# 256-token tiles at both ends of a fused token-mixing and two-layer kernel, with softmax by tile and weight pieces by order of need

## What is computed

```python
# x: (2, 4096, 192), weight_gen: (2, 4096, 8 heads, 7)
w = softmax(weight_gen, axis=-1)                      # 7 mixing weights for each token and head
x_pad = concat([zeros(B, 6, D), x], axis=1)           # causal window of 7 tokens
out[b, s, h, :] = sum_k w[b, s, h, k] * x_pad[b, s + k, h, :]
x = out.reshape(8192, 192)
x = (sigmoid(x @ w_gate) * (x @ w_val)) @ w_out1      # 192 -> 1536 -> 192
h = x @ w_in                                          # 192 -> 2048
P = a0 + a1*h + a2*h**2 + a3*h**3
Q = 1 + |b0|*|h| + |b1|*h**2
return (P / (Q + 1e-6)) @ w_out2                      # 2048 -> 192
```

## Time and profile before

| | before |
|---|---|
| median of three runs | 1456.27 us |
| the profiled execution, its own time | 1456.45 us |
| its span | 1454.7 us |
| PE busy | 1375.1 us (95%), 7040 matmuls |
| weight loads on PE | 1224.0 us (84%) |
| DVE busy | 1221.6 us (84%) |
| ACT busy | 1047.2 us (72%) |
| POOL busy | 356.3 us (24%) |
| moved by DMA | 36.22 MB, 25 GB/s in the mean |

### The profile page before, as it was taken

One profiled execution on the slowest core, in us unless ns is written; L12 is line 12 of the kernel. 1 busy time (PEld: TensorE's weight loads), 2 busy tenths in 40 slices (PEclk: granted clock), 3 DMA queues, 4 the chain that ended last, 5 costly groups with the idle time before them and its releaser, 6 DMA issues.

```text
span 1454.7 us, 18169 instructions
## 1 busy us (share of the span) xinstructions
PE 1375.1 (95%) x7040; PEld 1224.0 (84%) x7040; DVE 1221.6 (84%) x1327; ACT 1047.2 (72%) x1357; POOL 356.3 (24%) x204
## 2 busy tenths in 40 slices
PE   2679999999999999999999999999999999999876
PEld 1568889888989988898988889898888988898765
DVE  6554989888988988898898889889888988888898
ACT  3325877877777787777778777877877787787774
POOL 0534123231413323141332314132231423200000
PEclk9889999999999999999999999999999999999999
DMA  8410001001010100101010010101001010000000
GB/s 208 117 75 1 31 1 42 0 1 42 1 42 0 42 1 1 42 1 42 1 42 1 0 42 0 42 1 42 1 1 41 1 42 1 11 1 11 0 11 11
DMA packets 13103, 36.22 MB, mean 25 GB/s; under 512 B 1240, under 2 KB 6872, under 8 KB 12760
## 3 DMA queue, kind: packets, MB, share of 16 engines
q1 hardware_dynamic: 12952, 35.05, 8.2%
q0 software_dynamic: 64, 0.00, 0.0%
HBM read 27.16 MB, written 7.90 MB: 24 GB/s over the span
## 4 chain that ended last, share of the span: by engine, by line
PE 88%; DVE 8%; ACT 2%; issue 1%; DMA 1%; SPq 0%; ACTq 0%; DVEq 0%
PE ring L284 48%; PE acc L312 37%; DVE work L630 1%; DVE work L639 1%; DVE work L623 1%; PE ring L339 1%; DVE work L609 1%; PE ring L342 1%; DVE work L603 1%; DMA window<-in_x_dram 1%; DVE work L616 1%; DVE mixed L530 0%; DVE prod L525 0%; DVE in_w L566 0%; ACT work L433 0%
## 5 line engine op out<-in xcount | busy, mean ns | idle before, releaser
L312 PE MATMUL acc<-out_w,work 128*128 128x192 f32 x2048 | 371.4, 329 | 20.9 <-DVE work L639 17.8
L312 PEld LDWEIGHTS acc<-out_w,work 128*128 128x128 f32 x2048 | 342.4, 192 | 30.0 <-DVE work L639 21.1
L284 PE MATMUL ring<-yt,in_w 128*128 128x512 f32 x1280 | 321.8, 397 | 3.4 <-DVE work L609 1.7
L530 POOL TENSOR_TENSOR mixed<-mixed,prod 128x768 f32<-128x768 f32 x90 | 164.5, 1828 | 562.6 <-DVE work L616 412.2
L312 PE MATMUL acc<-out_w,u 128*128 128x192 f32 x1536 | 275.7, 330 | 19.5 <-DVE u L596 19.5
L284 PEld LDWEIGHTS ring<-yt,in_w 128*128 128x128 f32 x1280 | 240.4, 189 | 58.0 <-issue 2.1
L603 DVE TENSOR_TENSOR work<-ring,work 128x512 f32<-128x512 f32 x256 | 175.4, 685 | 130.1 <-ACT work L435 128.4
L312 PEld LDWEIGHTS acc<-out_w,u 128*128 128x128 f32 x1536 | 258.9, 192 | 26.8 <-DVE u L596 20.7
L284 PE MATMUL ring<-xt,gate_w 128*128 128x512 f32 x960 | 274.6, 416 | 4.6 <-DVE xt L577 4.6
L424 ACT ACTIVATE u<-ring 128x512 f32<-128x512 f32 x192 | 116.6, 608 | 211.5 <-PE ring L284 210.7
L284 PE MATMUL ring<-xt,val_w 128*128 128x512 f32 x960 | 257.3, 398 | 1.2 <-DVE u L596 1.2
(11 more groups left out here) (57 smaller groups left out, 869.5 us busy)
## 6 DMA issues: line engine op xcount, KB each, us to landing
window<-in_x_dram SPq DMA_DIRECT2D x14, 960.0 KB
out_dram<-zsb SPq DMA_DIRECT2D x16, 384.0 KB, 5.5
window<-in_x_dram SPq DMA_DIRECT2D x4, 472.5 KB
work<-in_weight_gen_dram SPq DMA_DIRECT2D x1, 1568.0 KB, 16.5
mix_weights<-work SPq DMA_DIRECT2D x1, 1568.0 KB, 5.1
mixw<-mix_weights SPq DMA_DIRECT2D x14, 112.0 KB
out_w<-in_moe_w_out_dram SPq DMA_DIRECT2D x1, 1536.0 KB, 23.2
out_w<-in_moe_w_out_dram SPq DMA_DIRECT2D x1, 1152.0 KB, 17.5
```

The source lines that it names most:

```text
L284: last = nc.tensor.matmul(dst[:, :], wt[:, c], xs[:, :], start=n == 0, stop=n == 4)
L312: last = nc.tensor.matmul(dst, src[:, n * P:(n + 1) * P], w[:, i, :], start=i == 0 and n % 2 == 0, stop=i == last_i and n % 2 == 1, skip_g ...
L530: engine.tensor_tensor(flat, flat, prod[:, :], ALU.add).then_inc(s_mix, 1)
```

## The change

Seventeen tiles take the place of sixteen: the first and the last hold 256 tokens, the fifteen others 512 (`BLOCKS`), so `NK` grows from 73 to 77, and every operation on a 256-token tile has half as many columns. The window of tile 0 is 8 rows and no longer waits for the zeroing; 4 more rows for tile 1 come in a load of their own behind the first eight pieces. POOL's mixing of tile 1 loses its waits by `slot`. The softmax of tiles 0 to 2 (560 elements a partition) is one part ahead of the first mixing; each later tile has its own (224 elements): reduce_max and subtract in quarter 4c-7, exp, sum, addition, reciprocal and product in quarter 4c-6 for tile c. The trip through DRAM goes. Weights come in 16 pieces of their own buffers: 256, 512 and 768 columns of w_gate and w_val, then 1024 and 1024 of w_in; 0 to 3 are split before quarter 0, 4 to 7 in quarter 0, 8 to 11 in quarter 1, 12 to 15 in quarters 2 to 4. in1 and in2 of the first tile wait only for the pieces that they read. In `QUARTER` the last out1 and out2 change places, and DVE takes cubic(n+1) ahead of quadratic(n+2).

```diff
-PIECE = 768
-BUFFERS = 12
-QUARTER = "21ab122bYbaab1X2"
+BLOCKS = [2] + [4] * 15 + [2]
+FIRST = 3
+QUARTER = "21ab122bYbaba1X2"
...
+    ROWS = HALO + OFFS[2]
+    def tokens(j):
+        return BLOCKS[j] * P
...
-        window = sb("window", [P, WIN])
-        mixw = sb("mixw", [P, CW])
+        window = sb("window", [P, ROWS, D])
+        mixw = sb("mixw", [P, FIRST * CW])
+        top = sb("top", [P, FIRST * J * H])
+        total = sb("total", [P, FIRST * J * H])
...
+        def weights(c):
+            return mixw[:, CW * (c % FIRST + 1) - BLOCKS[c] * HK:CW * (c % FIRST + 1)]
+        def soft_part(c):
+            return 0 if c < FIRST else c - FIRST + 1
+        pieces, at = [], 0
+        for layers, widths in ((((w_gate, gate_w), (w_val, val_w)), (256, 512, 768)), (((w_in, in_w),), (1024, 1024))):
+            c0 = 0
+            for n in widths:
+                for w, dst in layers:
+                    for kind, hi, lo in (("A", dst[0], dst[1]), ("B", dst[2], dst[2])):
+                        pieces.append((kind, w, c0, n, hi, lo, work[:, at:at + n]))
+                        at += n
+                c0 += n
+            assert all(w.shape[1] == c0 for w, _ in layers)
+        n_pieces = len(pieces)
...
+            def load_first_window():
+                rows = HALO + OFFS[1]
+                for b in range(B):
+                    p0, n = b * (P // B), P // B - 1
+                    sp.dma_start(window[p0:p0 + 1, HALO:rows, :], x_rows[p0:p0 + 1, 0:OFFS[1], :]).then_inc(s_window0, 16)
+                    at = (p0 + 1) * TP - HALO
+                    src = x_flat[at:at + (n - 1) * TP + rows, :]
+                    src = bass.AP(src.tensor, src.offset, [[TP * D, n], [1, rows * D]])
+                    sp.dma_start(window[p0 + 1:p0 + 1 + n, 0:rows, :].rearrange("p r d -> p (r d)"), src
+                                 ).then_inc(s_window0, 16)
+            def load_second_window():
+                sp.dma_start(window[:, HALO + OFFS[1]:ROWS, :], x_rows[:, OFFS[1]:OFFS[2], :]).then_inc(s_window1, 16)
             def load_window(c):
-                if c > 0:
-                    sp.wait_ge(s_mix, MIXES * c)
...
-            def load_soft(part):
-                lo, hi = parts[part]
-                sp.dma_start(softw[:, lo * CW:hi * CW], wg_rows[:, lo * CW:hi * CW]).then_inc(s_softw[part], 16)
+                sp.wait_ge(s_mix, MIXES * c)
+                sp.dma_start(window[:, 0:HALO + BLOCKS[c], :], x_rows[:, OFFS[c] - HALO:OFFS[c + 1], :]
+                             ).then_inc(s_window, 16)
+            def load_weights(c):
+                sp.wait_ge(s_mix, MIXES * (c - FIRST + 1))
+                sp.dma_start(weights(c), wg_rows[:, OFFS[c] * HK:OFFS[c + 1] * HK]).then_inc(s_weights[c % FIRST], 16)
...
-            load_soft(0)
-            sp.wait_ge(s_zero, B)
-            load_window(0)
+            sp.dma_start(mixw[:, FIRST * CW - OFFS[FIRST] * HK:FIRST * CW], wg_rows[:, 0:OFFS[FIRST] * HK]
+                         ).then_inc(s_weights[0], 16)
+            load_first_window()
             for n in range(8):
                 load_piece(n)
-            load_soft(1)
-            sp.dma_start(out1_w[:, :, :], w_out1.rearrange("(f p) d -> p f d", p=P)).then_inc(s_outw1, 16)
-            load_window(1)
-            load_soft(2)
-            for n in range(8, n_pieces):
+            load_second_window()
+            sp.dma_start(out1_w[:, 0:4, :], out1_rows[:, 0:4, :]).then_inc(s_outw1[0], 16)
+            for n in range(8, 12):
+                load_piece(n)
+            sp.dma_start(out1_w[:, 4:F1, :], out1_rows[:, 4:F1, :]).then_inc(s_outw1[1], 16)
+            for n in range(12, n_pieces):
                 load_piece(n)
             sp.dma_start(out2_w[:, :, :], w_out2.rearrange("(f p) d -> p f d", p=P)).then_inc(s_outw2, 16)
-            sp.wait_ge(s_soft, 18)
-            sp.dma_start(scratch[:, 2 * CW:], softw[:, 2 * CW:]).then_inc(s_scratch, 16)
-            sp.wait_ge(s_scratch, 16)
             for c in range(2, NCH):
+                if c + 1 < NCH and c + 1 >= FIRST:
+                    load_weights(c + 1)
...
-                if n == 0:
-                    pe.wait_ge(s_split, n_pieces)
-                    pe.wait_ge(s_scratch, 16)
-                first_product(bank("2", n), in_w, yt[j % 2], i).then_inc(s_h, 1)
+                if j == 0:
+                    pe.wait_ge(s_split, pieces_until(w_in, i * P))
...
-                    split_high(4)
-                    split_high(5)
-                    exponential(1)
-                    split_high(6)
-                    split_high(7)
+                    for c in range(4, 8):
+                        split_high(c)
+                if k == 1:
+                    for c in range(8, 10):
+                        split_high(c)
+                if k == 2:
+                    split_high(12)
+                if k == 3:
+                    split_high(13)
+                if k == 4:
+                    split_high(14)
+                if k % 4 == 2 and k > 5:
+                    exponential((k - 1) // 4 + 2)
...
                 sigmoid(m + 1)
                 if k == 1:
-                    exponential(2)
-                if k in (2, 3):
-                    for c in range(3 * k + 2, 3 * k + 5):
+                    for c in range(10, 12):
                         split_high(c)
+                if k == 4:
+                    split_high(15)
...
+                if c == 0:
+                    eng.wait_ge(s_window0, 32 * B)
+                    eng.wait_ge(s_zero, B)
+                elif c == 1:
+                    eng.wait_ge(s_window1, 16)
+                else:
+                    eng.wait_ge(s_window, 16 * (c - 1))
+                eng.wait_ge(s_soft, 6 * (soft_part(c) + 1))
...
-                    split_low(4)
-                    split_low(5)
-                    for step in range(6, 12):
-                        soft(step)
-                    split_low(6)
-                    split_low(7)
+                    for c in range(4, 8):
+                        split_low(c)
+                if k == 1:
+                    for c in range(8, 10):
+                        split_low(c)
+                if k == 2:
+                    split_low(12)
+                if k == 3:
+                    split_low(13)
+                if k == 4:
+                    split_low(14)
+                if k % 4 == 2 and k > 5:
+                    for step in range(2, 6):
+                        soft((k - 1) // 4 + 2, step)
...
                 gated(m + 1)
                 if k == 1:
-                    for step in range(12, 15):
-                        soft(step)
-                if k == 2:
-                    for step in range(15, 18):
-                        soft(step)
-                if k in (2, 3):
-                    for c in range(3 * k + 2, 3 * k + 5):
+                    for c in range(10, 12):
                         split_low(c)
+                if k == 4:
+                    split_low(15)
                 quadratic(n + 1)
                 denominator(p)
+                cubic(n + 1)
                 quadratic(n + 2)
-                cubic(n + 1)
+                if k % 4 == 1 and k > 4:
+                    for step in range(2):
+                        soft(k // 4 + 2, step)
                 cubic(n + 2)
...
             for c in range(1, NCH):
                 for k in range(MIXES):
-                    slot(c, k)
+                    if c > 1:
+                        slot(c, k)
                     mix(pool, nc.gpsimd, c, k)
```

More of the change, by code:

```diff
@@ L79, in bank @@
         def bank(u, i, half=0):
-            return ring[place[u, i, half] % BANKS]
+            j = i // F1 if u == "1" else i // F2 if u == "2" else i
+            return ring[place[u, i, half] % BANKS][:, 0:tokens(j)]
         gate_w = [sb(f"gate_w{n}", [P, F1 * P], F32R) for n in range(3)]
@@ L104, in moe_kernel, with slots, den, sqr @@
         qconst = sb("qconst", [P, 1])
[L109 to L125, removed]
+        def slots(at, count, j):
+            w = tokens(j)
+            if w == T or count == 1:
+                return work[:, at * T:at * T + (count - 1) * T + w]
+            return work[:, at * T:(at + count) * T].rearrange("p (n t) -> p n t", t=T)[:, :, 0:w]
+        def den(n, count=1):
+            return slots(n % 8, count, n // F2)
+        def sqr(n, count=1):
+            return slots(8 + n % 8, count, n // F2)
+        def num(n, count=1):
+            return slots(16 + n % (2 * NPAIRS), count, n // F2)
+        def u(m):
+            return u1[m % NU][:, 0:tokens(m // F1)]
+        def weights(c):
[13 more added lines that the diff above has]
+        n_pieces = len(pieces)
+        def pieces_until(w, at):
+            return max(n + 1 for n, p in enumerate(pieces) if p[1] is w and p[2] <= at < p[2] + p[3])
         s_coef = sem("coef_loaded")
@@ L382, in split_high, with exponential @@
             def split_high(n):
```

(16 more changed lines are left out.)

244 lines of the change are left out of this document (109 added, 135 removed).

## The result

The changed kernel took 1441.28 us (median of four runs, 1439.64 to 1442.0). The kernel before, on the same chip, took 1456.97 (1455.87 to 1458.01). The ratio is 0.9891 with a 95% interval of 0.9874 to 0.9908: 1.1% less time. The profiled span is 1440.2 us, where the sum gave 1439.

The account below looks back on a forecast made before the run. PE was taken to bound the middle and DVE the end. Start 63.5, quarters 4 to 11 133.1, middle 1102.4 and end 140 sum to a 1439 us span; with 1.75 more the forecast is 1441, its own range 1434 to 1448.

Parts of the forecast that it names:

- Window and softmax: Start: the 8-row window takes 6.8 us, mixing starts at 10.5 (bounds 8 and 12), softmax ends at about 9, hidden.
- Splits 4 to 7: Quarter 0: four weight splits on DVE, 0.69 us each plus waits for POOL of about 1.5 each, 7.9 us together.
- Quarter 4 at 63.5: End of the start: quarter 4 begins at 63.5 us, bounds 52 and 70; before it was 105.02.
- Quarters 4 to 11, 133.1: Stage 2 of tile 0 is half: 130.1 us plus 3 for fixed latencies; quarter 12 starts at 196.6.
- 57 ahead: Balance: 57 us ahead at quarter 12, 40.5 given back for four more quarters and the last tile's stage 2 alone.
- 52 steady quarters, 1102.4: Middle: 52 quarters of 21.2 us bring quarter 64 to 1299.
- 256-column matmuls at 0.125: Matmuls of the 256-token tiles on PE: 0.125 us each, between 0.116 and 0.162.
- rival C: 256-column matmuls aren't cheaper than 512-column ones: 24 us more, 1465 us; chance 4%.
- The end, 140: From quarter 64 on: quarters 64 to 67 at 16.8 us each, half quarters 8.7, sum 140 against 99.5 before.
- (A): Start: splits and POOL do not collide, 12 us of waits fall away, quarter 4 at 52 to 56: 1430 us; 17%.
- (B): Middle: softmax inside the quarters stalls PE beyond 2.6 us slack, 27 us more: 1467, 9%; smaller stall, 1445 to 1453, 8%.
- (D): Clock stays at 1.2 GHz in quarters 0 to 3 and 69 to 72: 7 us and 5 us more, 1453; 12%.

Follow-up runs that it names:

- exp_first: The changed kernel with the first exp and first four weight splits put ahead of ACT's wait for coef; 1438.01 us.
- hold_pad32: The changed kernel with the edits of exp_first and exp_hold, and an unused tile of 128 bytes a partition in front of top; 1425.14 us.
- exp_hold: exp_first with GpSimd's first mixing operation of tile 1 held until weight pieces 0 to 7 are split; 1435.73 us.
- dummy8: The changed kernel with eight added reduce_max of 224 elements on DVE behind the softmax steps, on an unused tile of 1920 bytes; 1454.41 us.
- all512: The changed kernel with BLOCKS back to sixteen tiles of 512 tokens, all else as changed; 1441.63 us.
- end_only: The changed kernel with BLOCKS of fifteen tiles of 512 tokens and then two of 256, so small tiles at the end only; 1448.64 us.

## Why the prediction was right, point by point

The forecast was 1441, and 1441.3 came. The steps, by their own numbers:

1. *Window and softmax: wrong.* "Mixing starts at 10.5" was 13.20, past its own bound of 12 and past the 13 that it named as a sign of failure. The step counted SP's issues and forgot what they were moved past: coef on POOL's queue, whose landing ACT waits for ahead of exp. "The softmax ends at about 9, hidden under it" was 13.06, and not hidden. exp_first brought mixing to 10.85, near the forecast; but in hold_pad32, with the same start, the window let mixing begin only at 12.65, so that the window's price came so close is partly luck.
2. *13 operations, copy, transposes, split: right.* 10.46 us from mixing to in1(0), forecast 10.6.
3. *Splits 4 to 7: right,* 7.64 us against 7.9, each about 1.2 us over its plain 0.70:

```profile
26.54 3.51 DVE L607 TENSOR_TENSOR gate_w<-work,gate_w 128x512 fp32r<-128x512 f32 x2
30.08 4.13 DVE L607 TENSOR_TENSOR val_w<-work,val_w 128x512 fp32r<-128x512 f32 x2
...
40.57 3.75 DVE L607 TENSOR_TENSOR gate_w<-work,gate_w 128x768 fp32r<-128x768 f32 x2
...
44.69 4.34 DVE L607 TENSOR_TENSOR val_w<-work,val_w 128x768 fp32r<-128x768 f32 x2
```

   Splits 8 to 11 took 8.1, forecast 9. PE's idle time behind them, forecast at 6 us:

```profile
34.72 1.65 PE L330 MATMUL acc<-out_w,u 128*128 128x192 f32 x4 [5.46 <-DVE u L637]
```

   exp_hold shows the mechanism by taking GpSimd away. The price of a split was mis-sized: "about 1.5" for each of 8 would be 12 us, and the waits were 9.1, 1.2 each for the splits of 512 and 1.06 for those of 768 (8.09 less 4 x 0.96).
4. *Quarter 4 at 63.5:* 65.5. The 2.7 of step 1, less 0.7 won elsewhere.
5. *Quarters 4 to 11, 133.1:* quarter 12 starts with five in2 ahead of its gate at 200.6, at 199.4, so 133.9. The 253.5 that the prediction has for quarter 12 of the kernel before was worked out and not read; the trace has 256.4. So the "57 ahead" came true because both ends of it were 2.8 to 2.9 us too early.
6. *52 steady quarters, 1102.4:* quarter 64 starts at 1298.8, so 1099.4, 21.14 each. The forecast had 1299, since the 3.0 less here met the 2.0 and 0.8 more of steps 4 and 5. That the sum is so close is partly luck.
7. *256-column matmuls at 0.125:* five take 0.60 from start to start, 0.12 each. This sank rival C.

```profile
1299.94 0.76 PE L303 MATMUL ring<-xt,gate_w 128*128 128x256 f32 x5
1300.54 0.76 PE L303 MATMUL ring<-xt,val_w 128*128 128x256 f32 x5
```

8. *The end, 140:* 141.4. Quarters 64 to 67 took 18.7, 16.7, 16.6 and 16.6 (forecast 16.8 each), half quarters 8.87 (8.7). The first, at 18.7, is the miss, and past the 18 that the prediction had named as another sign of being wrong. DVE was busy 89% of the last 55 us (48.7 us) and not 97%; up to its last operation, at 1435.8, it was 96%.

The rivals. (A), no collision, is excluded by the splits. (B), the softmax as a stall: its slack of 2.6 us was taken from a quarter of before; with the softmax steps in it, 1.6 to 1.8 are left, and nothing of the 29 us became due: PE shows no idle time between 200 and 1290. dummy8 shows that the mechanism is real from there on. exp did get a table load of its own, as the part on the middle allowed for (12 of 1.28 us between 200 and 1290), under cover. (D) stayed small: the granted clock was 0.83, 0.83 and 0.91 in the 20 us windows from 20, 40 and 60, and 0.91, 0.91, 0.83 in the three from 1380, so it stood at its lower level for a part of them only; the kernel before had 0.83, 0.74 and 0.83 from 40 to 100, and 0.91, 1.00, 0.91 in the same three. The sum carried 1.2 us for it at the start and nothing at the end.

One reading in the prediction was right in number and wrong in sense. "57 us ahead, 40.5 given back" (42.5 measured) treats the small tiles as the source of the gain with a price. all512 shows that they lead by 22 us at quarter 4 and return all of it, and that the rest of the change makes the 1.1%, between quarters 2 and 4. The prediction has no term that tells the two apart. A sum for one version can't show this; a second sum, for the change without its tiles, would have.

## What to carry to other kernels

When loads are moved forward on one queue, look at every small load on the other queues, and at what its waiter holds up: here a load of 1 KB held the exponential from 5.2 to 9.9 us. Shorter tiles at the ends pay only if the overlap they win isn't returned in extra steps; try the same change without them. And before a tuned matmul loop is judged, shift the tiles behind the weights by 128 bytes: it was worth 0.7% here, more than most edits, and an edit that changes the size of any tile can shift them unseen.

## What the runs showed of the hardware

- The placement of operands in SBUF changed the pace of the 512-column float32r matmuls: 0.227 us each with the rounded x at a multiple of 256 bytes, 0.233 with it 128 bytes beside one, in every kernel read. That made 10.3 us of 1441. The kernel before has the slower place too (0.233 and 21.15 us a quarter); it was not run at the faster one. The Trainium skill (TensorE: Matmul & The Clock Gate, Part 1) gives 215.7 ns from start to start for 512 columns with a warm array; neither pace here reaches that, and the page doesn't speak of placement.
- DVE with two SBUF inputs against GpSimd: four splits of 512 in 2.8 us alone and in 7.65 beside it. The Trainium skill (SBUF — State Buffer, two separate sides) says that the two take a shared port pair as an exclusive lock for a whole instruction. The trace agrees: an equal share of one bandwidth could stretch 0.70 to 1.40 at most (an estimate), and the mean here is 1.9.
- The addition of the softmax steps, 32 numbers a partition with one input, took 0.18 us at the start of the kernel before, and 0.65 to 0.94 inside the changed kernel. Each of the 14 long ones began while a GpSimd operation was under way and ended within 0.1 us behind it, as here; the sum ahead of it ran beside the same operation and kept its 0.37 to 0.39. In end_only the last one (16 numbers) met no GpSimd operation and took 0.17.

```profile
247.73 1.54 POOL L562 TENSOR_TENSOR prod<-window,mixw 128x768 f32<-128x768 f32 x1
...
248.65 0.65 DVE L595 TENSOR_SCALAR total<-total 128x32 f32<-128x32 f32 x1
```
